# A gated recurrence with two feed-forward layers: the forget gate by the logistic function instead of exponential, addition and reciprocal

## The reference

```python
sig = 1.0 / (1.0 + np.exp(-f_logit))
f = lower_bound + (1.0 - lower_bound) * sig
for t in range(S):                       # S = 6080
    h = f[:, t] * h + (1.0 - f[:, t]) * x[:, t]
    y[:, t] = h
h1 = y @ w_in0                           # 256 -> 2048
z = (h1 / (1.0 + np.exp(-1.702 * h1))) @ w_out0
h2 = z @ w_in1
g = np.where(h2 >= 1, h2, np.where(h2 <= -1, 0.0, (h2 + 1) ** 2 / 4))
return g @ w_out1
```

## Time and profile before

| | us |
|---|---|
| median of 3 runs | 1019.85 |
| lowest, highest | 1019.74, 1020.58 |
| the profiled execution | 1019.84 |
| its span, first to last instruction | 1018.0 |

### The profile page before, as it was taken

The page is one execution under the profiler, slowest core; times in us unless marked ns, Lnnn a source line. Parts: engine busy times, 40 slices in busy tenths (PEclk is TensorE's granted clock), DMA queues, the critical chain, the costliest instruction groups (busy, mean ns, idle before and its releaser), DMA issues.

```text
span 1018.0 us, 14275 instructions
## 1 busy us (share of the span) xinstructions
PE 1007.9 (99%) x4401; PEld 821.9 (81%) x4401; DVE 752.0 (74%) x1050; ACT 720.4 (71%) x1336; POOL 578.6 (57%) x473
## 2 busy tenths in 40 slices
PE   7999999999999999999999999999999999999998
PEld 5988988888888888888888888888888888888886
DVE  8978767786577896668898767889665556767676
ACT  8766777666777777777678677768766667777665
POOL 4567867757567365356647446655635664573432
PEclk9999999999999999999999999999999999999999
DMA  8775574436523222442323333232323222232421
GB/s 287 239 241 203 193 245 165 155 125 209 205 94 107 74 99 84 161 145 73 108 74 105 132 113 138 73 109 73 109 73 137 87 78 104 73 110 72 147 76 42
DMA packets 53212, 130.76 MB, mean 128 GB/s; under 512 B 6032, under 2 KB 16912, under 8 KB 52112
## 3 DMA queue, kind: packets, MB, share of 16 engines
q1 hardware_dynamic: 53136, 129.85, 36.5%
HBM read 106.82 MB, written 23.00 MB: 128 GB/s over the span
## 4 chain that ended last, share of the span: by engine, by line
PE 98%; DVE 1%; DMA 0%; issue 0%; ACT 0%; DVEq 0%
PE chain L562 26%; PE acc L606 17%; PE acc L603 17%; PE acc L602 17%; PE pair L562 13%; PE single L562 8%; DVE gate L1133 1%; DMA gate<-f_logit_dram 0%; DVE state L1165 0%; DVE state L1146 0%; DVE zout L1245 0%; ACT gate L767 0%; ACT gate L765 0%; DVE xin0lo L1202 0%; DVEq L1164 0%
## 5 line engine op out<-in xcount | busy, mean ns | idle before, releaser
L1497 POOL TENSOR_TENSOR g_lo<-g_act,g_hi 128x512 fp32r<-128x512 f32 (+1 forms) x269 | 361.5, 1345 | 398.6 <-ACT g_hi L913 394.5
L873 ACT ACTIVATE spare<-chain 128x512 f32<-128x512 f32 x240 | 143.1, 596 | 179.5 <-PE chain L562 178.7
L1257 DVE TENSOR_TENSOR spare<-pair,spare 128x512 f32<-128x512 f32 x160 | 109.8, 686 | 147.3 <-PE pair L562 146.7
L913 ACT ACTIVATE g_hi<-g_act 128x512 fp32r<-128x512 f32 (+1 forms) x269 | 168.0, 625 | 9.6 <-DVE g_act L1281 7.4
L562 PE MATMUL chain<-xin1hi,w_main 128*128 128x512 f32 x416 | 162.5, 395 | 0.0
L606 PE MATMUL acc<-g_lo,w_down0hi 128*128 128x512 f32 (+1 forms) x384 | 150.2, 391 | 0.0
L606 PE MATMUL acc<-g_lo,w_down1hi 128*128 128x512 f32 (+1 forms) x384 | 150.1, 391 | 0.0
L603 PE MATMUL acc<-g_hi,w_down1lo 128*128 128x512 f32 (+1 forms) x384 | 149.9, 390 | 0.0
L603 PE MATMUL acc<-g_hi,w_down0lo 128*128 128x512 f32 (+1 forms) x384 | 149.9, 390 | 0.0
L602 PE MATMUL acc<-g_hi,w_down0hi 128*128 128x512 f32 (+1 forms) x384 | 149.8, 390 | 0.0
L602 PE MATMUL acc<-g_hi,w_down1hi 128*128 128x512 f32 (+1 forms) x384 | 149.7, 390 | 0.0
(11 more groups left out here) (129 smaller groups left out, 2041.4 us busy)
## 6 DMA issues: line engine op xcount, KB each, us to landing
w_main<-sums_kept SPq DMA_DIRECT2D x80, 512.0 KB, 3.7
w_main<-blocks_kept SPq DMA_DIRECT2D x80, 256.0 KB, 2.9
w_a<-blocks_kept SPq DMA_DIRECT2D x80, 128.0 KB, 3.9
blocks_kept<-w_main SPq DMA_DIRECT2D x16, 512.0 KB, 4.0
w_main<-blocks_kept SPq DMA_DIRECT2D x16, 512.0 KB, 3.3
sums_kept<-xin0hi SPq DMA_DIRECT2D x16, 512.0 KB, 2.9
zout<-w_in_dram SPq DMA_DIRECT2D x24, 256.0 KB, 4.4
out_dram<-zout SPq DMA_DIRECT2D x10, 512.0 KB, 5.3
```

The source lines that it names most:

```text
L873: act.activation(snap[k][:, 0:n], chain[g % 2][:, 0:n], ACT.Copy).then_inc(s_snap, 1)
L913: act.activation(g_hi[h % 4][:, 0:n], activated(h), ACT.Copy).then_inc(s_ghi, 1)
L1257: dve.tensor_tensor(to[:, 0:n], bank[:, 0:n], snap[(0, 2, 1)[k]][:, 0:n], ALU.add).then_inc(s_evac, 1)
L1497: pool.tensor_tensor(g_lo[h % 4][:, 0:n], g_act[h % 4][:, 0:n], g_hi[h % 4][:, 0:n].bitcast(F32), ALU.subtract).then_inc(s_glo_pool, 1)
```

## The change

ScalarE's logistic function of minus the logit takes the place of exponential, addition and VectorE's reciprocal, and the factor is f = 1 + (lb-1) x sigmoid(-logit). In chunk 0 VectorE makes the factors of parts 0 and 1, ScalarE those of 2 and 3. The four low parts of chunk 0 are all VectorE's. The first up block is loaded from ScalarE's queue, the other first loads are issued by SP in another order. TensorE's first matmuls take two tiles together, channel half by channel half. The steps of later chunks stand at other tiles and groups. The number of 224-, 448- and 512-column matmuls is the same.

```diff
 SP: the first loads
-            for q in range(K):
-                load_first(gate, f_logit, part_columns(0, q)[0], s_gate_first[q])
+            load_first(gate, f_logit, part_columns(0, 0)[0], s_gate_first[0])
             sp.dma_start(lb[:], lower_bound).then_inc(s_lb, 16)
-            load_raw_up(0, 0)
             load_first(state, x, half(0), s_x_first[0])
+            load_first(gate, f_logit, part_columns(0, 1)[0], s_gate_first[1])
+            load_raw_up(0, 1)
             load_first(gate, f_logit, half(1), s_gate_early[1])
             load_first(state, x, half(1), s_x_first[1])
-            load_raw_up(0, 1)
             load_raw_down(0, 0)
+            load_raw_up(0, 2)
             load_raw_down(0, 1)
+            load_raw_up(0, 3)
             sp.dma_start(gate[:, 1024:2048], ...)
             sp.dma_start(state[:, 1024:2048], ...)
-            load_raw_up(0, 2)
-            load_raw_up(0, 3)
 TensorE
+            def first_up(h, s):
+                n = WIDTH[0] // 2
+                cols = slice(h * n, (h + 1) * n)
+                if s % 2 == 0:
+                    for k in range(K):
+                        pe.wait_ge(s_first_lo, 2 * h + k + 1)
+                        mm = up(0, s, cols, (k,))
+                        if k == 0:
+                            up(0, s + 1, cols, (0,))
+                    return mm
+                return up(0, s, cols, (1,))
...
-            pe.wait_ge(s_rec, 1)
+            pe.wait_ge(s_sigmoid, 1)
             for _ in range(9):
                 pe.matmul(pair[:], warm[:, 0:P], warm[:], start=True, stop=True)
 ScalarE
-                act.activation(part, part, ACT.Exp, scale=-1.0).then_inc(s_exp, 1)
-                act.activation(part, part, ACT.Copy, bias=1.0).then_inc(s_inc, 1)
+                act.activation(part, part, ACT.Sigmoid, scale=-1.0).then_inc(s_sigmoid, 1)
...
-                act.activation(factors(c, q), gate[:, cols], ACT.Identity, bias=lb[:, k:k + 1],
-                               scale=one_less_lb[:, k:k + 1]).then_inc(s_f, 1)
+                act.activation(factors(c, q), gate[:, cols], ACT.Identity, bias=1.0,
+                               scale=lb_less_one[:, k:k + 1]).then_inc(s_f, 1)
...
-            first_piece()
-            for q in range(2):
-                exp_step(0, q)
-                inc_step(0, q)
+            act.dma_start(raw_up[0], up_source[0][0]).then_inc(s_raw_up[0], 16)
+            sigmoid_step(0, 0)
+            sigmoid_step(0, 1)
             blocks_hi(0, 0)
-            f_step(0, 0)
-            f_step(0, 1)
-            exp_step(0, 2)
-            inc_step(0, 2)
+            sigmoid_step(0, 2)
             first_hi(0)
-            exp_step(0, 3)
-            inc_step(0, 3)
+            f_step(0, 2)
+            blocks_hi(0, 1)
             first_hi(1)
-            blocks_hi(0, 1)
-            for q in range(2, 4):
-                f_step(0, q)
+            sigmoid_step(0, 3)
+            f_step(0, 3)
+            first_hi(2)
             down_hi(0, 0)
-            first_hi(2)
-            exp_step(1, 0)
             first_hi(3)
-            inc_step(1, 0)
             down_hi(0, 1)
 ScalarE, plain stage 0 and the groups of layer 1
+                    if s in (2, 4):
+                        sigmoid_step(1, s // 4)
+                    if s in (3, 5):
+                        f_step(1, s // 5)
...
+                    if g % 2 == 0:
+                        sigmoid_step(c + 1, g // 2)
+                    else:
+                        f_step(c + 1, g // 2)
 VectorE, groups of layer 1
-                if place > 0 and l == 0 and c + 1 < CHUNKS and g >= 1:
-                    recurrence(c + 1, 3 * (g - 1) + place - 1)
+                if l == 0 and c + 1 < CHUNKS:
+                    if g % 2 == 1 and place == 3:
+                        drive_step(c + 1, g // 2)
+                    if g in (2, 4, 6) and place == 1:
+                        scan_step(c + 1, g // 2 - 1)
 VectorE, the start
-            for h in range(2):
-                for q in (2 * h, 2 * h + 1):
-                    reciprocal_step(0, q, 0)
-                    reciprocal_step(0, q, 1)
-                for q in (2 * h, 2 * h + 1):
-                    drive_step(0, q)
-                    scan_step(0, q)
-            first_lo(2)
-            first_lo(3)
+            first_f(0)
+            first_f(1)
+            drive_step(0, 0)
+            scan_step(0, 0)
+            drive_step(0, 1)
+            first_lo(0)
+            scan_step(0, 1)
+            drive_step(0, 2)
+            first_lo(1)
+            scan_step(0, 2)
+            drive_step(0, 3)
+            first_lo(2)
+            scan_step(0, 3)
+            first_lo(3)
             keep_carry(0)
 GpSimd, the start
             blocks_lo(0, 0)
-            first_lo(0)
-            first_lo(1)
             blocks_lo(0, 1)
-            pool.wait_ge(s_first_lo_dve, 2)
+            pool.wait_ge(s_first_lo, 4)
             down_lo(0, 0)
             down_lo(0, 1)
```

## The result

| | before | after |
|---|---|---|
| median of 22 runs, us | 1019.82 | 1021.75 |
| lowest to highest | 1019.68 to 1020.58 | 1019.05 to 1022.52 |
| the profiled execution | 1019.84 | 1021.38 |
| its span | 1018.0 | 1019.6 |
| VectorE, ScalarE busy in the span | 752.0, 720.4 | 686.8, 705.2 |

The ratio is 1.0016, interval 1.001 to 1.0023. The changed kernel is 1.9 us slower, less than the 2.04 us that the prediction took as the border, but its interval leaves 1 out. The forecast of 1018.7 missed, and 1021.75 lies 1.15 us above the upper end of the range. Its executions also scatter more: one of the 22 took 1019.05, the others 1020.72 to 1022.52.

The account below looks back on a forecast made before the run. TensorE, busy 99% of 1018.0 us, was taken as the bound, so only its start counts: 2.0 us sooner by the input, cut to 1.15 by the first block's store. 1019.84 - 1.15 = 1018.7, range 1017.4 to 1020.6.

Parts of the forecast that it names:

- Rival 2: TensorE's clock stays or falls low in the thinner start, costing 1.4 to 2.0 us: 1019.6 to 1020.4; chance 0.12.
- rival 1: The first block's store doesn't bind, so the full 2.0 us is gained: 1017.8; chance 0.18, half counted as faster.
- before's gap of 1.0 us did no harm: TensorE's gap before 13.61 us in the kernel before, taken as evidence against a low clock after the change.
- by the input alone everything behind would come 2.0 us sooner: TensorE's start: tile 0's last matmul at 12.4 us instead of 14.40, so all behind it 2.0 us sooner.
- T: Landing of the second half's gate values, head of the start's chain: 6.9 + 0.86 - 0.85 = 6.9 us.
- head start: Time won by the first block's load from ScalarE's queue: 0 to 1.05 us, taken as 0.85.
- The second low part: One of four low parts in the start's chain from T, each counted at 0.38 us.
- What is left of the chain: Second half's sigmoid to the fourth low part's end: 5.2 us from T, ready at 12.1.
- The store: ScalarE's third block step waits for the first block's store, landing about 15.3 instead of 16.1; gain limited to 1.1 to 1.15 us.
- The rest is worth nothing: Behind the start, ScalarE's 22 additions and VectorE's 88 reciprocals saved gain nothing; earlier factor steps and drives cost nothing.
- Rival 3: Sigmoid and tanh need different activation tables, two loads of 2.57 us per sigmoid behind the start: 1030; chance 0.04.

Follow-up runs that it names:

- the mended kernels: After with matmuls on ones filling TensorE's gaps, warm-ups released by the second sigmoid, or either with GpSimd's split held back: medians 1019.47 to 1019.98 us.

## Why the prediction was wrong

**The case named second was the true one.** Rival 2, TensorE's clock, had a chance of 0.12. 21 of the 22 executions of after lie above 1020.7; eleven of them have it in the record of the clock, and that the other ten have it too rests on the runs that mend it. The price given for it, 1.4 to 2.0 us, was right as a total: 1.4 to 1.5 us in the trace, about 2 us between the two courses. Its parts were not: it was to be 36 matmuls at 0.187 us, and the trace has 15 distances of 0.213. Nor was it added to the right base, for with this price the forecast of 1018.7 gives 1020.1 to 1020.7, and not 1019.6 to 1020.4. (A smaller slip: half of rival 1's 0.18 is 0.09, where the chance of faster was given as 0.12.) What tipped the weight was the sentence that before's gap of 1.0 us did no harm. The rows that it needed were in view: before had one idle time behind the warm-ups, after was to have two in a row with six matmuls between them, and rows 8 told when the warm-ups are released and when they end. The prediction had even written that they end by 7.4 with the real work near 8.0. The Trainium skill (TensorE: Matmul & The Clock Gate, HAM oscillation — how this bites in real kernels) tells of bursts of matmuls that are parted by waits and so run at half clock. After's trace agrees in kind only: the granted clock was 0.50 behind two such waits, though it fell within the second burst, not ahead of it. The prediction hadn't weighed it.

**The base of the sum was too good.** The step that failed is "by the input alone everything behind would come 2.0 us sooner"; it came 0.1 sooner. It failed in three terms, and even with the clock up the forecast of 1018.7 would have been missed.
- T. Forecast 6.9, with a head start of 0.85. In after's trace the load took longer than in before:

```profile
L489 SPq DMA_DIRECT2D gate<-f_logit_dram x1: 432/432/432, 3.1 to 3.1; - x1
...
DMA to landing us min/median/max: 4.8/4.8/4.8
```

  3.1 + 4.8 = 7.9, one us later than rows 4. In the eight profiled executions with after's loads and steps the second half's sigmoid starts between 6.81 and 7.88, 7.3 on average, against 6.92 and 7.06 in the two with after's steps and before's loads. So the head start for the small packets was 0.4 on average, and the spread of 1.1 us belongs to the new order. The transfers did start fuller, as argued (273 GB/s in 2.70 to 4.10 instead of 151), but on average the gate's small packets got only half of it.
- The second low part. Forecast 0.38 from rows 7, whose two low parts ran on VectorE beside no GpSimd step; measured 1.08. The prediction put all four on VectorE and left out that GpSimd's step on the second block would now run beside them. That is 0.7 us.
- What is left of the chain: from the sigmoid's start to the end of the fourth low part 6.0 us instead of 5.2, of which 0.7 is the second term. The fourth low part ended at 13.92 instead of 12.1, before's at 14.03: 0.1 us sooner, not 2.

**The store.** Forecast landing 15.3. In after:

```profile
L428 SPq DMA_DIRECT2D blocks_kept<-w_main x1: 331/331/331, 8.1 to 8.1; - x1
DMA to landing us min/median/max: 6.7/6.7/6.7
```

8.1 + 6.7 = 14.8, which is 1.3 us sooner than in rows 9. That is one execution against one: over all traces the store lands at 14.7 to 15.4 in the nine with the new loads (15.1 on average) and at 15.4 to 16.1 in the five with the old ones (15.8). The head start is thus 0.7 us and the forecast of 15.3 was close. The mechanism was right, but it didn't bind in after: ScalarE's third block step starts at 17.71, late for another reason. It bound in the kernel with the logistic function alone. So the store didn't bind, as rival 1 has it, but the gain that rival 1 hung on this did not come, since nothing else was early.

**The rest is worth nothing.** Right in that it wins nothing. From the first down product to the last matmul it is 997.25 us before, and 997.1 to 997.9 in all executions with the change's later steps. But it can cost: at the second chunk's first matmul, where GpSimd's low part ends just before it, after lost 0.3 us in its first trace and nearly 0.5 in its second. The list of waits shows only the second case (0.24 us). VectorE's 65 us are won for nobody.

**The table.** Rival 3 fell. The groups of ScalarE in after, 0 to 14 us:

```profile
L781 ACT ACT_TABLE_LOAD x1 | 1.3, 1283 | 1.2 <-PEq L1570 1.2
```

It is the only load in the kernel.

**What stays open.** Without the low clock the change is worth nothing that was measured: the medians of the mended kernels with its loads (1019.47 to 1019.98) lie from 0.35 us below to 0.08 above before in the same group, and no interval leaves 1 out. The better course of after has its first down product at 15.83, 0.8 us sooner than before, and yet took 1019.74: 0.65 us went behind it, nearly 0.5 of it at 47.2 to 47.5 us and 0.2 near 131. The wait for GpSimd explains the first place; the second is not explained. Nor is it settled why one execution of the same program keeps its clock and the next doesn't. The landing of the gate values alone is not it: it was 6.98 in after's better execution and 7.88 in the worse, but 6.92 in the run with the old loads, where the clock was low, and 7.70 with the late warm-ups, where it was high.

## What to carry to other kernels

When a change speeds up the producer of an event that releases the warm-up matmuls, look at where the warm-ups end against the first real matmul: hang them on a later event so that they run up to the data, which here cost one digit and no work; too late an event holds the first real matmul back. Price a low clock by where it lies, since in a stretch that ends in a wait it is free and on the unbroken row of matmuls each one takes nearly double (0.213 us instead of 0.112). And when a step is moved to another engine, its duration is that of its new neighbours: list what the other engines do beside it.

## What the runs showed of the hardware

In after's first trace the clock fell to half 4 us behind the end of nine warm-ups, though no idle time of TensorE behind them was over 1.1 us, and stayed low for 3.3 us of unbroken matmuls; in its second, with idle times of 0.2 and 0.9 us, it did not fall. The granted clock can read 1.00 while 224-column matmuls are 0.213 us apart, as in the runs with the old loads (8.2 to 15.0 us) and with four warm-ups (up to 12.6), in both before any real matmul had run at the high level; at that level they are 0.112 apart. A VectorE subtraction of two SBUF operands, 0.39 us alone, took 1.08 us beside a GpSimd instruction of 1.27 us, and 1.28 us in the kernel with before's loads. With the first block issued by ScalarE's queue and the other loads in the new order, the first block's store landed 0.7 us sooner on average, and the second half's gate values, in small packets, between 0.1 us sooner and 1.0 later.
